# Attention and experts in one kernel: products in two parts, x taken a step later, two weight loads ahead of two stores, and ScalarE in place of GpSimd for the high parts of k

## The chip, the cores and the metric

One core of one Trainium2 chip runs one program. The metric is the device time of one execution in microseconds (us), as the median of several. Engines are named as in the profile: PE (TensorE matmul) and PEld (its weight loads), DVE (VectorE), ACT (ScalarE), POOL (GpSimd), SP (SyncE, which here issues nearly every DMA; SPq is its queue).

## The reference

Attention over 2 batches, 8 heads, 576 positions, head width 64, with a bias that a small network of the relative position gives, and then a layer of 4 experts (512 to 1024 to 512) over the 1152 rows that come out.

```python
# attention, for each batch and head
scores = (q @ k.T) / sqrt(64)
x      = log1p(|i - j|) / log1p(max(i, 1))
bias   = relu(x[..., None] @ w1 + b1) @ w2          # 32 hidden units, one bias per head
attn   = exp(scores + bias - rowmax)
attn   = attn / (sum(attn) + 1e-9)
x_attn = attn @ v
# experts
p   = domain_probs / (sum(domain_probs) + 1e-9)
out = sum over e of p[:, e] * (relu(x_attn @ W1[e]) @ W2[e])
```

## The kernel before

Matmuls whose accuracy matters are done on a high and a low part of each operand: hi is a copy of the fp32 value rounded to a shorter type, lo is the rest, and PE adds three products (hi·hi, hi·lo, lo·hi). So each operand costs two elementwise instructions ahead of PE.

The work runs in this order.

- **Bias of blocks 0 to 15** (EARLY = 16). For each block of 16 query rows DVE and ACT make the hidden layer (hidden_of_block, lines 689 to 700 and 855 to 865), PE sums it (sum_block, L988 to L1003), ACT scales it (scale_block, L867 to L874), and SP stores it to DRAM (store_rows, L480 to L483).
- **Pass 0 of attention**: the first 256 query rows, for PAIRS = 8 pairs of heads, with two steps of 128 rows for each pair. Step s of 16 is ORDER0[s] = (p, t); from step 4 on, step 2p is (p, 0) and step 2p + 1 is (p, 1). For a step PE makes scores (score_step, L1031), DVE adds the bias and takes the row maximum (add_bias, L723), ACT makes exponentials (exponents, L890), DVE inverts the sums (invert, L735 and L738), POOL scales the rows (normalise, L647), PE transposes them two steps later (turn, L1060 and L1064; LAG = 2), and ACT (turns 0, 2 and 4 of a pair) and DVE (turns 1 and 3) copy the transposed blocks out (take_turn, L896 and L743). There are two transposition banks; a turn waits until the turn two before it has been copied out. When both steps of a pair are transposed, PE multiplies by v (products, L1089; 20 matmuls), at the steps that PRODUCTS_AT names: step 5 for pair 0, 6 for pair 1, 2p + 4 for pairs 2 to 6. ACT and DVE then take the result x out in a high and a low part (high_of_x L901, low_of_x L748), in the same step and behind that step's take_turn. All x of pass 0 go through one PSUM bank, x_bank.
- **q and k**: POOL also makes the high and low parts of each pair's k and q (high_of_qk L619 and L623 in odd steps, low_of_qk L633 and L637 in even ones), three pairs ahead. SP reloads qk_raw when they are done.
- **The turn to the experts**: behind pass 0, PE runs hidden_part(0, 0), the last turns, hidden_part(0, 1), the products of pair 7, sum_block(16), hidden_part(0, 2) and sum_block(17). Of these hidden parts three of four contraction slices run at once, the last one after x of pair 7 is there. Then a table of positions (POS = 16 for each expert) weaves experts and the rest: hidden_part(0, 3) at position 3, then sum_block(18) and (19), and so on; the bias blocks 18 to 35 lie at positions 3 to 11.
- **Weights**: 64 chunks of 512 KB. Chunk n goes into w_raw slot n % 2 (load_chunk, L489 to L501, which waits until chunk n - 2 has its low part), ACT makes its high part (high_of_chunk, L912) and DVE its low part (low_of_chunk, L754). Chunks 0 and 1 are loaded in pass 0. At position 0, 1 and 2 of the first expert each of ACT and DVE first takes the hidden bank (L919, L761) and then chunk 2, 3 and 4; **at position 2 both make the hidden layer of bias blocks 18 and 19 behind chunk 4.** SP's list there is: store_rows(16), store_rows(17), load_chunk(2), load_chunk(3), and at position 0 load_chunk(4).
- **Pass 1 of attention** (the other 320 rows) is woven into the experts of the first half of the rows, and experts over the second half follow.

Every engine runs its own fixed list in order; semaphores tie them together. The order of the lists above is written out by hand.

Of the kernel before, what the change touches and what calls it, by code (L numbers as in the profile page):

```python
# [24 lines left out]
JT = 5  # L25
# [28 lines left out]
LAG = 2  # L54

# [12 lines left out]
PRODUCTS_AT = {5: 0, 6: 1, **{2 * p + 4: p for p in range(2, PAIRS - 1)}}  # L68
# [129 lines left out]
def bank_place(n):  # L198

    if n < WOVEN_FROM:  # L200
        return (3, 0, 1)[n % 3]
    if n < WOVEN_END:
        return 2 + n % 2
    return n % 4
# [6 lines left out]
def attention_and_experts(nc, qk_t, v, b_w, probs_in, w1, w2,  # L211
# [3 lines left out]
    with ExitStack() as top:  # L215
# [70 lines left out]
        qk_split, scored, maxed, exped = (sem(s) for s in ("qk_split", "scored", "maxed", "exped"))  # L286
        plus_eps, recip_done, normed = (sem(s) for s in ("plus_eps", "recip_done", "normed"))
# [39 lines left out]
        def split_count(g):  # L327

            return SPLITS[0] * min(g + 1, PAIRS) + SPLITS[1] * max(0, g + 1 - PAIRS)
# [45 lines left out]
        def x_place(f):  # L375

            if f == 0:
                return x_bank[:, 0:ROWS0].rearrange("p (c q) -> p c q", c=2)
            return score_bank[0][:, :, HALF:HALF + ROWS1 // 2]
# [42 lines left out]
        def free_bank(eng, n):  # L422

            if n < 3:
                eng.wait_ge(maxed, blk(0, PAIRS - 1, 3) + 1)
            if n == WOVEN_FROM:
                eng.wait_ge(x_lo_out, PAIRS)
            if n >= WOVEN_END and bank_place(n) < 2 and n < WOVEN_END + 4:
                eng.wait_ge(maxed, blk(1, PAIRS - 1, 4) + 1)
            if bank_before(n) is not None:  # L430
                bank_taken(eng, bank_before(n))

        with nc.Block() as block:

            @block.sync
            def _(sp):
# [85 lines left out]
                for p in range(PAIRS):  # L522
# [10 lines left out]
                    if p == 6:  # L533
                        sp.dma_start(p_raw[:, 0:2, :], probs_in[0:ROWS0, :].rearrange("(t p) e -> p t e", p=P)
                                     ).then_inc(p_in, 16)
                        sp.dma_start(p_raw[:, 2:4, :], probs_in[S:S + ROWS0, :].rearrange(
                            "(t p) e -> p t e", p=P)).then_inc(p_in, 16)
                        sp.dma_start(p_raw[:, 4:6, :], probs_in[ROWS0:4 * P, :].rearrange(
                            "(t p) e -> p t e", p=P)).then_inc(p_in, 16)
                        sp.dma_start(p_raw[0:D, 6, :], probs_in[4 * P:S, :]).then_inc(p_in, 16)  # L540
                        sp.dma_start(p_raw[D:P, 6, :], probs_in[S + ROWS0:S + ROWS0 + D, :]).then_inc(p_in, 16)
                        sp.dma_start(p_raw[:, 7:9, :], probs_in[S + ROWS0 + D:N, :].rearrange(
                            "(t p) e -> p t e", p=P)).then_inc(p_in, 16)
                store_rows(EARLY)
                store_rows(EARLY + 1)
                load_chunk(2)
                load_chunk(3)
# [49 lines left out]
            def _(pool):  # L597
# [14 lines left out]
                def high_of_qk(g):  # L612
# [6 lines left out]
                    pool.tensor_scalar(kh, k_raw, 1.0, 1.0, ALU.mult, ALU.mult).then_inc(qk_split, 1)  # L619
# [8 lines left out]
                def low_of_qk(g):  # L628
# [3 lines left out]
                    pool.wait_ge(qk_split, split_count(g) - len(pieces) - 1)  # L632
                    pool.tensor_tensor(kl, k_raw, kh.bitcast(F32), ALU.subtract).then_inc(qk_split, 1)  # L633
# [40 lines left out]
            def _(dve):  # L674
# [70 lines left out]
                def low_of_x(f, p):  # L745
                    n = PAIRS * f + p
                    dve.wait_ge(x_hi_out, n + 1)
                    dve.tensor_tensor(x_slice(x_lo, f, p), x_place(f), x_slice(x_hi, f, p).bitcast(F32),  # L748
# [29 lines left out]
                for s in range(STEPS + LAG):  # L778
# [4 lines left out]
                    if 1 <= s <= STEPS:  # L783
                        invert(0, *ORDER0[s - 1])
                    if s >= LAG:
                        p, t = ORDER0[s - LAG]
                        take_turn(0, p, 2 * t + 1)
                    if s in PRODUCTS_AT:
                        low_of_x(0, PRODUCTS_AT[s])
                    if s == STEPS - 1:  # L790
                        low_of_chunk(0)
                    if s == STEPS:
                        hidden_of_block(EARLY)
                        low_of_chunk(1)
                hidden_of_block(EARLY + 1)
# [52 lines left out]
            def _(act):  # L848
# [43 lines left out]

                def take_turn(f, p, i):
# [4 lines left out]
                def high_of_x(f, p):  # L898
                    n = PAIRS * f + p
                    act.wait_ge(weighed, n + 1)  # L900
                    act.copy(x_slice(x_hi, f, p), x_place(f)).then_inc(x_hi_out, 1)  # L901
# [19 lines left out]
                for s in range(STEPS + LAG):  # L921
# [3 lines left out]
                    if s < STEPS:  # L925
                        q, u = ORDER0[s]
                        exponents(0, q, 2 * u)
                        exponents(0, q, 2 * u + 1)
                    if s >= LAG and t == 1:
                        take_turn(0, p, 4)  # L930
                    if s in PRODUCTS_AT:
                        high_of_x(0, PRODUCTS_AT[s])
                    if s == STEPS - 1:
                        high_of_chunk(0)
                    if s == STEPS:
                        hidden_of_block(EARLY)
                        high_of_chunk(1)
                hidden_of_block(EARLY + 1)
# [48 lines left out]
            def _(pe):  # L987
# [24 lines left out]
                def score_step(f, p, t):  # L1012
# [5 lines left out]
                    elif f == 1 and p == 0 and t == 0:  # L1018
                        pe.wait_ge(scaled, BLOCKS)
                        for n in range(WOVEN_FROM - 2, WOVEN_FROM):  # L1020
# [49 lines left out]
                def products(f, p):  # L1070
# [5 lines left out]
                    if n >= 1:  # L1076
                        pe.wait_ge(x_lo_out, n)
# [5 lines left out]
                    to = x_place(f)  # L1083
                    for c in range(chunks):
                        for t in range(JT):
                            for side in range(2):
                                half = slice(D * side, D * side + D)
                                dst = x_bank[half, 0:width] if f == 0 else to[half, c, :]
# [3 lines left out]
                    mm.then_inc(weighed, 1)  # L1092
# [44 lines left out]
                for s in range(STEPS + 1):  # L1137
# [6 lines left out]
                    if s in PRODUCTS_AT:  # L1144
                        products(0, PRODUCTS_AT[s])

# [88 lines left out]
```

## Time and profile before

| what | value |
|---|---|
| median of 3 runs | 620.22 us (620.11 to 623.03) |
| the profiled execution, own time | 620.98 us |
| its span in the trace | 619.2 us |
| PE busy | 578.6 us (93%) |
| DVE, ACT, POOL busy | 295.3, 263.4, 121.7 us |
| DMA | 72.72 MB, mean 117 GB/s |
| mean granted PE clock | 0.978 of full |

Busy time is the sum of an engine's instructions without overlaps. The span is about 1.8 us shorter than the execution's own time. The chain of work that ended last is 83% PE. A row of the timeline gives start, duration, engine, line, operation, tiles, how many instructions were merged, and in brackets how long the engine had been idle before and who ended that.

### The profile page before, as it was taken

To read this page: it belongs to the slowest core of one execution; us is meant where nothing else is said; L and a number is where in the kernel's file an instruction comes from. 1 tells how busy PE (TensorE), PEld (TensorE's weight loads), DVE (VectorE), ACT (ScalarE), POOL (GpSimd) and SP (SyncE) were. 2 spreads that over 40 slices of the span, in tenths; PEclk is the share of its full clock that TensorE was granted. 3 is DMA by queue.
4 is the path that set the end of the run, shared out by engine and by line. 5 is a ranking of instruction groups with operands and counts; after the bars stand their busy time and mean duration, and the time that the engine had idled before them with its cause. 6 is when DMAs were issued, how large, how long until landed. Compare 5 with 4: busy or idle time off the path is not lost.

```text
span 619.2 us, 9781 instructions
## 1 busy us (share of the span) xinstructions
PE 578.6 (93%) x3864; PEld 466.7 (75%) x3864; DVE 295.3 (48%) x608; ACT 263.4 (43%) x506; POOL 121.7 (20%) x176
## 2 busy tenths in 40 slices
PE   3857998949999999999999999999999999999997
PEld 1345666526677888878878788998899889989986
DVE  7935667377646633464245624261255226224511
ACT  4845666357535644464336534352045015303400
POOL 5136689000001141324313331000000000000000
PEclk9868999969999999999999999999999999999999
DMA  5882565357355552173164301241223114221201
GB/s 153 227 308 79 168 196 140 107 154 223 115 168 171 171 147 92 44 238 122 47 179 125 124 35 53 85 154 34 69 73 131 35 34 137 69 69 52 85 35 51
DMA packets 60654, 72.72 MB, mean 117 GB/s; under 512 B 23232, under 2 KB 39872, under 8 KB 60608
## 3 DMA queue, kind: packets, MB, share of 16 engines
q1 hardware_dynamic: 60416, 72.08, 38.3%
q8 instruction: 31, 0.51, 0.3%
q14 instruction: 15, 0.12, 0.1%
q10 hardware_dynamic: 192, 0.01, 0.0%
HBM read 59.10 MB, written 12.98 MB: 116 GB/s over the span
## 4 chain that ended last, share of the span: by engine, by line
PE 83%; DVE 4%; DMA 4%; ACT 4%; issue 2%; POOL 2%; ACTq 0%; DVEq 0%; SPq 0%; POOLq 0%
PE m_bank L1126 12%; PE scores L1109 11%; PE x_bank L1126 11%; PE scores L1126 10%; PE m_bank L1109 9%; PE x_bank L1109 9%; PE turn L1060 4%; PE scores L1031 4%; PE scores L1089 4%; PE x_bank L1089 3%; PE scores L999 3%; PE turn L999 2%; POOL probs L647 2%; DVE hidden L699 2%; ACT w_hi L912 1%
## 5 line engine op out<-in xcount | busy, mean ns | idle before, releaser
L647 POOL TENSOR_SCALAR probs<-probs,recip 128x576 f32<-128x576 f32 x72 | 53.0, 746 | 242.8 <-DVE recip L738 242.5
L754 DVE TENSOR_TENSOR w_lo<-w_raw,w_hi 128x1024 fp32r<-128x1024 f32 x64 | 79.8, 1246 | 29.8 <-ACT w_hi L912 29.8
L723 DVE CUSTOM_DVE_ANT_0 probs<-scores,bias 128x576 f32<-128x576 f32 x72 | 52.0, 755 | 47.7 <-PE scores L1031 33.8
L896 ACT COPY probs_t<-turn 128x512 f32<-128x512 f32 (+2 forms) x80 | 42.4, 552 | 69.7 <-PE turn L1060 68.5
L912 ACT CAST w_hi<-w_raw 128x1024 fp32r<-128x1024 f32 x64 | 66.5, 1046 | 7.3 <-DMA w_raw<-w_in 7.3
L890 ACT ACTIVATE probs<-probs,neg_max 128x576 f32<-128x576 f32 x72 | 55.4, 772 | 27.4 <-DVE neg_max L723 27.3
L1060 PE MATMUL turn<-ident,probs 128*128 128x128 f32 x288 | 45.2, 286 | 5.2 <-POOL probs L647 5.0
L1109 PE MATMUL scores<-x_hi,w_hi 128*128 128x384 f32 (+2 forms) x148 | 47.9, 324 | 0.0
L1109 PE MATMUL scores<-x_lo,w_hi 128*128 128x384 f32 (+2 forms) x148 | 47.3, 320 | 0.0
L1109 PE MATMUL scores<-x_hi,w_lo 128*128 128x384 f32 (+2 forms) x148 | 47.3, 319 | 0.0
L1109 PE MATMUL m_bank<-x_hi,w_hi 128*128 128x512 f32 (+2 forms) x124 | 44.7, 361 | 0.2 <-DVE h_lo L761 0.2
L1060 PEld LDWEIGHTS turn<-ident,probs 128*128 128x128 f32 x288 | 32.9, 143 | 15.1 <-POOL probs L647 9.2
L1109 PE MATMUL m_bank<-x_hi,w_lo 128*128 128x512 f32 (+2 forms) x124 | 43.3, 349 | 0.0
L1109 PE MATMUL m_bank<-x_lo,w_hi 128*128 128x512 f32 (+2 forms) x124 | 43.1, 348 | 0.0
L919 ACT ACTIVATE h_hi<-scores 128x384 fp32r<-128x384 f32 (+2 forms) x37 | 15.3, 414 | 58.1 <-PE scores L1109 58.1
L1109 PE MATMUL x_bank<-x_hi,w_hi 128*128 128x512 f32 (+2 forms) x112 | 39.6, 353 | 0.0
L1126 PE MATMUL m_bank<-w_hi,h_hi 128*128 128x512 f32 x96 | 39.0, 406 | 0.0
L919 ACT ACTIVATE h_hi<-x_bank 128x512 fp32r<-128x512 f32 (+2 forms) x28 | 13.3, 477 | 59.9 <-PE x_bank L1109 59.9
L1109 PE MATMUL x_bank<-x_lo,w_hi 128*128 128x512 f32 (+2 forms) x112 | 38.5, 344 | 0.0
L1109 PE MATMUL x_bank<-x_hi,w_lo 128*128 128x512 f32 (+2 forms) x112 | 38.5, 344 | 0.0
L1126 PE MATMUL m_bank<-w_hi,h_lo 128*128 128x512 f32 x96 | 37.6, 391 | 0.0
L1126 PE MATMUL m_bank<-w_lo,h_hi 128*128 128x512 f32 x96 | 37.5, 390 | 0.0
(138 smaller groups left out, 1243.3 us busy)
## 6 DMA issues: line engine op xcount, KB each, us to landing
w_raw<-w_in SPq DMA_DIRECT2D x64, 512.0 KB, 3.7
qk_raw<-qk_t_in SPq DMA_DIRECT2D x16, 576.0 KB, 4.7
bias<-bias_scratch SPq DMA_DIRECT2D x16, 576.0 KB, 4.9
v<-v_in SPq DMA_DIRECT2D x32, 128.0 KB, 3.6
bias_scratch<-probs SPq DMA_DIRECT2D x13, 288.0 KB, 4.2
bias_scratch<-probs_t SPq DMA_DIRECT2D x10, 288.0 KB, 3.0
bias_scratch<-rows SPq DMA_DIRECT2D x8, 288.0 KB, 4.5
out_dram<-acc SPq DMA_DIRECT2D x8, 256.0 KB, 2.0
```

Source lines behind the costliest of these rows:

```text
L647: pool.tensor_scalar(tile, tile, recip[:, stat(f, p, j)], 1.0, ALU.mult, ALU.mult).then_inc(normed, 1)
L723: dve.tensor_tensor_reduce(probs_of(f, p, j).rearrange("p (c j) -> p c j", c=2), score_of(f, j)[:, :, 0:HALF], bias_of(f, p, j).rearrange( ...
L754: dve.tensor_tensor(lo, raw, hi.bitcast(F32), ALU.subtract).then_inc(w_lo_out, 1)
L890: act.activation(tile, tile, ACT.Exp, scale=-1.0, bias=neg_max[:, stat(f, p, j)], accum_out=row_sum[:, stat(f, p, j)]).then_inc(exped, 1)
L896: act.copy(sub_out(f, p, i), sub_in(n, i)).then_inc(out_act, 1)
L912: act.copy(hi, raw).then_inc(w_hi_out, 1)
L919: act.activation(hi, bank[:, cols], ACT.Relu).then_inc(hidden_hi, 1)
L999: mm = pe.matmul(sum_bank(n)[C * quad:C * quad + C, c, 0:HALF], w2_block[:, :, :].rearrange("p g h -> p (g h)"), hidden(n, quad)[:, HALF * ...
L1060: mm = pe.transpose(bank[:, P * t:P * t + P], probs_of(f, p, j)[:, P * t:P * t + P], ident[:, :])
L1089: mm = pe.matmul(dst, v_sb[:, 2 * (n % 2) + side, t, :], probs_t_of(f, p)[:, side, t, cols * c:cols * c + cols], start=t == 0, stop=t == J ...
L1109: mm = pe.matmul(m_bank(n)[:, 0:width], w, x, start=k == 0 and part == 0, stop=k == MT - 1 and part == 2)
L1126: mm = pe.matmul(m_bank(n), h, w[:, ft, :], start=ft == 0 and part == 0, stop=ft == FT - 1 and part == 2)
```

## The change

- PRODUCTS_AT now gives parts. For pairs 2 to 5 the products of contraction tiles 0 to 2 (12 matmuls) run in step 2p + 4 and those of tiles 3 and 4 (8 matmuls) in step 2p + 5. Pair 1 is split over steps 6 and 7. Pair 0 (step 5) and pair 6 (now at s = 16) run both parts together.
- x is taken out one step after the last part (X_AT). In DVE's list low_of_x stands ahead of that step's take_turn, in ACT's list high_of_x stands behind the exponentials and ahead of the copy of turn 4. Two PSUM banks take turns for x (last_bank for even pairs, x_bank for odd ones), so products wait for the x of the pair before the previous one; the order in which hidden and output tiles take banks is rotated.
- For pairs 3 to 7 (ON_ACT) the high part of k is an ACT copy in odd steps 3, 5, 7, 9 and 11, behind the exponentials and ahead of turn 4's copy; POOL's low part waits for it (k_high).
- SP's list has load_chunk(2) and load_chunk(3) ahead of store_rows(16) and store_rows(17).
- Chunk 0 is split at s = 16 and chunk 1 at s = 17, both before the hidden layer of blocks 16 and 17 and behind the turns of those steps. Before, chunk 0 was at s = 15, and chunk 1 at s = 16.

```diff
+ON_ACT = range(3, PAIRS)
...
-PRODUCTS_AT = {5: 0, 6: 1, **{2 * p + 4: p for p in range(2, PAIRS - 1)}}
+
+PART_T = ((0, 3), (3, JT))
+PRODUCTS_AT = {5: [(0, 0), (0, 1)], 6: [(1, 0)], 7: [(1, 1)],
+               **{2 * p + 4 + part: [(p, part)] for p in range(2, PAIRS - 2) for part in range(2)},
+               STEPS: [(PAIRS - 2, 0), (PAIRS - 2, 1)]}
+X_AT = {s + 1: p for s, parts in PRODUCTS_AT.items() for p, part in parts if part == 1}
...
-        return (3, 0, 1)[n % 3]
+        return (0, 1, 3)[n % 3]
...
-            return SPLITS[0] * min(g + 1, PAIRS) + SPLITS[1] * max(0, g + 1 - PAIRS)
+            return sum((SPLITS[o >= PAIRS]) - (o in ON_ACT) for o in range(g + 1))
...
-        def x_place(f):
+        def x_place(f, p):
 
             if f == 0:
-                return x_bank[:, 0:ROWS0].rearrange("p (c q) -> p c q", c=2)
+                return (last_bank, x_bank)[p % 2][:, 0:ROWS0].rearrange("p (c q) -> p c q", c=2)
...
+            if n == 2:
+                eng.wait_ge(x_lo_out, PAIRS - 1)
...
+                load_chunk(2)
+                load_chunk(3)
                 store_rows(EARLY)
                 store_rows(EARLY + 1)
-                load_chunk(2)
-                load_chunk(3)
...
-                    pool.tensor_scalar(kh, k_raw, 1.0, 1.0, ALU.mult, ALU.mult).then_inc(qk_split, 1)
+                    if g not in ON_ACT:
+                        pool.tensor_scalar(kh, k_raw, 1.0, 1.0, ALU.mult, ALU.mult).then_inc(qk_split, 1)
...
+                    if g in ON_ACT:
+                        pool.wait_ge(k_high, g - ON_ACT[0] + 1)
...
+                    if s in X_AT:
+                        low_of_x(0, X_AT[s])
                     if s >= LAG:
                         p, t = ORDER0[s - LAG]
                         take_turn(0, p, 2 * t + 1)
-                    if s in PRODUCTS_AT:
-                        low_of_x(0, PRODUCTS_AT[s])
-                    if s == STEPS - 1:
-                        low_of_chunk(0)
-                    if s == STEPS:
-                        hidden_of_block(EARLY)
-                        low_of_chunk(1)
-                hidden_of_block(EARLY + 1)
+                    if s >= STEPS:
+                        low_of_chunk(s - STEPS)
+                        hidden_of_block(EARLY + s - STEPS)
...
+                def high_of_k(g):
+                    act.wait_ge(raw_in[g % 2], 16 * (g // 2 + 1))
+                    act.wait_ge(scored, last_block_of(before_in_place(g)) + 1)
+                    act.copy(k_of(g)[0], qk_raw[:, g % 2, 1, :]).then_inc(k_high, 1)
...
+                    if s in X_AT:
+                        high_of_x(0, X_AT[s])
+                    if s % 2 and 3 + (s - 3) // 2 in ON_ACT:
+                        high_of_k(3 + (s - 3) // 2)
                     if s >= LAG and t == 1:
                         take_turn(0, p, 4)
-                    if s in PRODUCTS_AT:
-                        high_of_x(0, PRODUCTS_AT[s])
-                    if s == STEPS - 1:
-                        high_of_chunk(0)
-                    if s == STEPS:
-                        hidden_of_block(EARLY)
-                        high_of_chunk(1)
-                hidden_of_block(EARLY + 1)
+                    if s >= STEPS:
+                        high_of_chunk(s - STEPS)
+                        hidden_of_block(EARLY + s - STEPS)
...
-                def products(f, p):
+                def products(f, p, part=None):
+
                     n = PAIRS * f + p
                     on_act, on_dve = taken_by(f, p)
                     pe.wait_ge(out_act, on_act)
                     pe.wait_ge(out_dve, on_dve)
                     pe.wait_ge(v_in[n % 2], 48 * (n // 2 + 1))
-                    if n >= 1:
-                        pe.wait_ge(x_lo_out, n)
+                    if n >= 2:
+                        pe.wait_ge(x_lo_out, n if f else n - 1)
+                    first_t, end_t = (0, JT) if part is None else PART_T[part]
...
-                        for t in range(JT):
+                        for t in range(first_t, end_t):
                             for side in range(2):
                                 half = slice(D * side, D * side + D)
-                                dst = x_bank[half, 0:width] if f == 0 else to[half, c, :]
+                                dst = to[half, :, :] if f == 0 else to[half, c, :]
                                 mm = pe.matmul(dst, v_sb[:, 2 * (n % 2) + side, t, :],
                                                probs_t_of(f, p)[:, side, t, cols * c:cols * c + cols],
                                                start=t == 0, stop=t == JT - 1)
-                    mm.then_inc(weighed, 1)
+                    if end_t == JT:
+                        mm.then_inc(weighed, 1)
...
+                    for p, part in PRODUCTS_AT.get(s, ()):
+                        products(0, p, part)
```

## Rows read from the trace of the kernel before

**Rows 1.** The page: span, busy by engine, and one group (mean ns behind busy us).

```profile
span 619.2 us, 9781 instructions
PE 578.6 (93%) x3864; PEld 466.7 (75%) x3864; DVE 295.3 (48%) x608; ACT 263.4 (43%) x506; POOL 121.7 (20%) x176
...
L890 ACT ACTIVATE probs<-probs,neg_max 128x576 f32<-128x576 f32 x72 | 55.4, 772 | 27.4 <-DVE neg_max L723 27.3
```

**Rows 2.** What PE waited for, 38 to 142 us: total, times, longest.

```profile
PE scores L999 <- DVE probs L699: 9.7, 1, 9.7
...
PE turn L1064 <- ACT probs_t L896: 2.0, 6, 0.3
```

**Rows 3.** The chain that ended last, 104 to 136 us: start, duration, what.

```profile
107.62 0.60 PE turn L1064 x4
...
112.60 1.11 PE scores L999 x16
...
115.97 1.15 PE turn L999 x16
...
118.51 4.03 DMA w_raw<-w_in
...
124.89 3.57 DMA w_raw<-w_in
...
128.48 1.05 ACT w_hi L912
...
130.79 1.30 DVE probs L699 x3
...
132.22 2.15 PE scores L999 x16
134.37 1.79 PE turn L999 x16
```

**Rows 4.** Windows of 1 us: engines' busy time (instructions), granted clock, DMA.

```profile
49.00:50.00 1.00, 0.00 (x0) 0.00 (x0) 0.97 (x5) 1.00 (x4) 0.12 (x1) 1.00 0.00 0
...
122.00:123.00 1.00, 0.57 (x3) 0.15 (x1) 0.00 (x0) 0.44 (x1) 0.00 (x0) 1.00 0.94 365
...
125.00:126.00 1.00, 0.00 (x0) 0.00 (x0) 1.00 (x2) 0.88 (x2) 0.00 (x0) 0.83 0.03 10
...
135.00:136.00 1.00, 1.00 (x12) 0.22 (x4) 1.00 (x4) 0.17 (x1) 0.00 (x0) 0.55 0.00 0
```

**Rows 5.** The timeline, 98 to 119 us: all engines.

```profile
100.45 1.38 PE L1060 MATMUL turn<-ident,probs 128*128 128x128 f32 x8 [1.02 <-POOL probs L647]
...
101.66 1.23 DVE L754 TENSOR_TENSOR w_lo<-w_raw,w_hi 128x1024 fp32r<-128x1024 f32 x1 [1.68 <-ACT w_hi L912]
...
104.93 3.23 DVE L699 TENSOR_SCALAR probs<-table,shift 128x576 f32<-128x576 f32 x3
...
118.10 0.60 ACT L919 ACTIVATE h_hi<-m_bank 128x512 fp32r<-128x512 f32 x1 [0.21 <-PE m_bank L1109]
```

**Rows 6.** The timeline, 74 to 79.3 us: steps 9 and 10 of pass 0.

```profile
74.09 0.37 ACT L901 CAST x_hi<-x_bank 128x256 fp32r<-128x256 f32 x1 [0.86 <-PE x_bank L1089]
...
74.96 1.09 PE L1060 MATMUL turn<-ident,probs 128*128 128x128 f32 x8
...
77.67 0.57 ACT L896 COPY probs_t<-turn 64x512 f32<-64x512 f32 x1
...
77.90 1.32 PE L1060 MATMUL turn<-ident,probs 128*128 128x128 f32 x8
...
78.48 0.67 POOL L619 TENSOR_SCALAR k_hi<-qk_raw 128x576 fp32r<-128x576 f32 x1
...
78.56 0.42 PEld L1060 LDWEIGHTS turn<-ident,probs 128*128 128x128 f32 x4 [0.24 <-POOL probs L647]
```

**Rows 7.** The chain that ended last, 66 to 84 us: one pair of pass 0.

```profile
71.73 2.31 PE x_bank L1089 x20
...
79.22 2.31 PE x_bank L1089 x20
```

More of the change, by code:

```diff
@@ L286, in attention_and_experts @@
         qk_split, scored, maxed, exped = (sem(s) for s in ("qk_split", "scored", "maxed", "exped"))
+        k_high = sem("k_high")
         plus_eps, recip_done, normed = (sem(s) for s in ("plus_eps", "recip_done", "normed"))
@@ L747, in low_of_x @@
                     dve.wait_ge(x_hi_out, n + 1)
-                    dve.tensor_tensor(x_slice(x_lo, f, p), x_place(f), x_slice(x_hi, f, p).bitcast(F32),
+                    dve.tensor_tensor(x_slice(x_lo, f, p), x_place(f, p), x_slice(x_hi, f, p).bitcast(F32),
                                       ALU.subtract).then_inc(x_lo_out, 1)
@@ L900, in high_of_x @@
                     act.wait_ge(weighed, n + 1)
-                    act.copy(x_slice(x_hi, f, p), x_place(f)).then_inc(x_hi_out, 1)
+                    act.copy(x_slice(x_hi, f, p), x_place(f, p)).then_inc(x_hi_out, 1)
                 def high_of_chunk(n):
@@ L1019, in score_step @@
                         pe.wait_ge(scaled, BLOCKS)
-                        for n in range(WOVEN_FROM - 2, WOVEN_FROM):
+                        for n in range(WOVEN_FROM - 3, WOVEN_FROM):
                             bank_taken(pe, n)
@@ L1082, in products @@
                     cols = width // chunks
-                    to = x_place(f)
+                    to = x_place(f, p)
                     for c in range(chunks):
-                        for t in range(JT):
+                        for t in range(first_t, end_t):
                             for side in range(2):
                                 half = slice(D * side, D * side + D)
-                                dst = x_bank[half, 0:width] if f == 0 else to[half, c, :]
+                                dst = to[half, :, :] if f == 0 else to[half, c, :]
                                 mm = pe.matmul(dst, v_sb[:, 2 * (n % 2) + side, t, :],
@@ L1143, in _ @@
                         turns_of_step(*ORDER0[s - LAG])
-                    if s in PRODUCTS_AT:
-                        products(0, PRODUCTS_AT[s])
+                    for p, part in PRODUCTS_AT.get(s, ()):
+                        products(0, p, part)
                 def slot(at):
```

## Prediction

> **What bounds the kernel now.** I read four views, in this order. The page says that PE is busy for 578.6 of 619.2 us, so at most some 40 us lie outside its matmuls, and a change to the order of lists can only win there [rows 1]. The waits of PE in the stretch that the change touches say where: one single wait of 9.7 us ahead of sum_block(18), for the hidden layer that DVE makes at L699. Beside it the waits inside the pairs of pass 0 are small, 2.0 us in all for turn 4, which waits for the copy of turn 2 [rows 2]. The chain that ended last shows what stands in front of the 9.7 us: the load of chunk 2 is issued at 118.51, behind the second of two stores, lands at 122.54, its low part is done at 124.87, only then chunk 4 is issued, lands at 128.46, is split into high part (1.05) and low part until 130.79, and then DVE makes the hidden layer (1.30) and PE starts again at 132.22 [rows 3]. The windows of 1 us show the second price of the wait: PE's last work ends at about 122.57, its granted clock falls from full (2.4 GHz) to half (1.2 GHz) at about 125.7, 3.1 us later, and rises again at about 135.9, some 3.7 us after PE is back [rows 4].
>
> **The two loads ahead of the two stores.** This is the large term. load_chunk(2) waits for chunk 0's low part alone, which before is done at 102.9 [rows 5], so the load can be issued some 15 us earlier, at about 104, and lands by 108. load_chunk(3) waits for chunk 1's low part, which I put at 111 below; the stores behind it wait for ACT's scaling of block 16, which can't come before its sum ends at 113.7 [rows 3], so the queue is free for them and the move past them costs nothing. That cover is 2.7 us wide; a later chunk 1 would hold back both stores, which nobody near needs.
> With chunk 2 present, ACT takes it as soon as it has taken the first hidden bank: 118.10 + 0.60 [rows 5] + 1.05 for the cast [rows 3] + 0.02 + 1.23 for DVE's low part [rows 5] = 121.00, where it was 124.87. Chunk 4 is issued then, and everything behind it keeps its length: 3.57 load, 1.05, 1.23, 1.30 hidden layer [rows 3, 5]. DVE's other work there (the second and third hidden bank, as wide as ACT's copy of 0.60 [rows 5], and chunk 3's 1.23) fits into the 4.6 us between 121.0 and 125.6, since chunk 3 has landed by 115. So sum_block(18) starts 3.9 us earlier, at 128.3, and the wait is 5.8 us and not 9.7. What is late next is chunk 4 itself, because its slot is free only when chunk 2 is split. Bounds: the load took 3.57 once and 4.03 once [rows 3], so -3.9 or -3.4. Everything behind 132 is one engine's work in order and moves along: chunks 5 and 6 shift by the same 3.9 us.
>
> **The clock behind the wait.** The two sums behind it take 2.15 + 1.79 = 3.94 us at half clock; the same two sums take 1.11 + 1.15 = 2.26 us at full clock [rows 3]. The low clock costs 1.7 us. With 5.8 us without work and a fall seen 3.1 us after the stop I expect it to fall again and to cost the same: 0. A wait of about 1.7 us around 49 left it at full clock [rows 4], so the bounds are -1.7 (it stays high) and +1.7 (the low stretch is twice as long).
>
> **Pass 0, the pairs.** PE does the same matmuls in another order. An even step loses 8 of the 20 products to the odd step behind it; 20 take 2.31 us [rows 7], so 0.92 us moves. The wait of turn 4 for the copy of turn 2 stays (the turns stand next to each other as before). What can be won: in even steps from 8 on the second turn waits for POOL's row scaling, so that 8 transpositions take 1.32 us, against 1.09 in odd steps [rows 6]: 0.23 us in each of 4 steps, 0.9 us in all. With 0.92 us more work between odd scores and the even step's turns, POOL is ready in time, and that wait goes. What is late next is ACT. The second turn of an even step needs the copy of turn 4, which before ended at 78.24, 0.33 us ahead of 78.56 where that turn ran [rows 6]. Now the products give it 0.92 us more, and it is set back by the k copy and by DVE, whose turn copy now stands behind x. The k copy on ACT does not exist in the trace; 128x576 exponentials take 0.77 [rows 1] and the 128x1024 cast 1.05 [rows 3], a 64x512 copy 0.57 [rows 6]. I take 0.67, nearest to the row of equal width without its bias and sum. DVE: x comes behind two exponentials and ACT's 0.37 copy [rows 6]; by my laying out of the step, DVE reaches the next odd scores 0.5 us late. Slack: 0.33 + 0.92 - 0.67 - 0.5 = 0.1 us, about what there was for POOL. So in the three even steps behind a k copy (8, 10, 12) nothing is won, and in step 14 some 0.2 us. Bounds: -0.9 (all four) and +1.3 (k copy 1.0 us, three to four times).
> GpSimd loses 0.67 us per pair for pairs 3 to 7 [rows 6]. It has that slack in the middle of the pass, so this alone is worth 0 there. In the turns of pair 7 PE does wait for it, 1.02 us at 100.45 [rows 5]; the pairs there (8, 9) keep their k on POOL, and it starts that stretch about 0.3 us earlier.
>
> **The end of pass 0.** Chunk 0 is split one step later. ACT must copy turn (7, 0), copy x of pair 5 and cast chunk 0 (about 0.6 + 0.37 + 1.05), then DVE needs 1.23: together 3.25 us behind the first turn, against 0.66 for the second turn and 2.31 for the products [rows 7] on PE, 2.97. So of the 0.3 to 0.5 us by which that turn comes earlier, hidden_part(0, 0) keeps about 0.1 to 0.2. Chunk 1 is cast behind turn 4's copy of pair 7: 107.62 + 0.60 [rows 3] + 0.57 + 1.05 + 1.23 = 111.1; hidden_part(0, 2), which needs it, runs at 113.7. The wait for last_bank and the rotated banks hit free banks. Sum for all of pass 0: -0.2 us, with bounds -1.0 and +1.7.
> A row shows one danger here: three DVE instructions at 104.93 took 3.23 us beside POOL's work, while three of the same shape take 1.30 with POOL idle [rows 5, 3]. Chunk 0's low part took 1.23 at 101.66 [rows 5] and now falls at about 102.8, beside POOL's row scaling. The Trainium skill ("SBUF — State Buffer", section "Who interferes with whom") has a rule that speaks against the move: a VectorE instruction with two SBUF inputs and a GpSimd instruction that reads SBUF share one port pair, and the one that is issued second fully blocks. By that rule chunk 0's low part could stand behind one scaling of 0.73 us and hidden_part(0, 0) would start about 0.4 us later, and the sum would end at 616.5. The 3.23 us agree with it.
>
> **The sum.** -3.9 (load), 0 (clock), -0.2 (pass 0) = -4.1 us. The profiled execution took 620.98 us, so its counterpart would take 616.9 with a span of 615.1. The median of the runs, 620.22, is 0.76 below that one execution; the same 4.1 us off it gives 616.1.
>
> **The rivals.**
> 1. The clock stays high, because the wait is 4 us shorter. For it: 1.7 us at 49 didn't lower it [rows 4]. Against: 5.8 us is well over the 3.1 us after which it fell. It gives 616.1 - 1.7 = 614.4.
> 2. The clock comes back later, after some 7 us and not 3.7: 616.1 + 1.7 = 617.8.
> 3. Pass 0 wins its full 0.9 us and the earlier turn of pair 7 holds: 616.1 - 0.7 - 0.3 = 615.1.
> 4. The loads aren't early, or something else ends the wait at 132 (the change doesn't do what it says). For it: DVE's order at position 2 is unchanged, hidden layer behind chunk 4. Against: every link of the chain back to the store is a load or a split of a chunk [rows 3]. It gives 620.22 - 0.2 = 620.0.
> 5. On the other side: ACT sets the pace of pass 0. The place is a pair's odd step, where k copy (0.67), x copy (0.37) and DVE's x (0.42) all stand in one ring, scores to exponentials to x to the turn copy to the next scores. Where they lie in series and nothing hides them, each of the 5 pairs gains 1.46 us, 7.3 in all: 616.1 + 7.3 = 623.4. It decides against the change from 0.8 us per pair on, since 5 x 0.8 uses up the 4.1. Against it: a pair takes 7.49 us (79.22 - 71.73) [rows 7], ACT's work for one is 4 x 0.77 + 3 x 0.57 + 0.37 + 0.67 = 5.8, and it sat idle for 0.86 us ahead of x alone [rows 6].
>
> **How the numbers follow.** Forecast 616.1: 0.60. Rival 1: 0.14. Rival 2: 0.07. Rival 3: 0.08. Rival 4: 0.06. Rival 5: 0.05. A measurement of this kernel tells about 0.5% (3.1 us) from no change. Faster by over that (below 617.1) are rivals 1 and 3 and the forecast but for some 0.05 at its late end: 0.77. Within: rivals 2 and 4, that 0.05 and part of rival 5, 0.19. Slower: 0.04. The range takes in rivals 1 and 3 and the forecast's own bounds (load +0.5, pass 0 +1.7) and reaches to rival 2: 613.8 to 618.4.
>
> **What the next profile shows.** The large term is right if chunk 2's load is issued at about 104, ACT's cast of it stands directly behind the first hidden bank's copy, chunk 4 is issued near 121 and sum_block(18) waits under 6 us. It is wrong if PE's wait there still is 9 us. The clock term is read in the windows behind it: half clock for 3 to 4 us more of work. The term of pass 0 is right if a pair still takes about 7.5 us and an even step's 8 transpositions take 1.1 to 1.3 us; if turns wait for ACT's copy of turn 4 by more than 0.3 us each, rival 5 has come in part. The forecast falls if PE waits for more than 3 us in all behind 140 us, where now it is busy nearly throughout.

## The result and the profile after

| what | before | after |
|---|---|---|
| median | 622.55 us (7 runs, 620.11 to 623.26) | 618.31 us (7 runs, 617.07 to 619.85) |
| ratio to before | | 0.9945 (0.993 to 0.996) |
| profiled execution, own time / span | 620.98 / 619.2 us | 618.14 / 616.3 us |
| PE's wait ahead of sum_block(18) | 9.65 us | 5.91 us |
| PE, DVE, ACT, POOL busy | 578.6, 295.3, 263.4, 121.7 us | 580.0, 295.9, 265.9, 117.9 us |

The change makes the kernel 0.55% faster, with 0.4 to 0.7% in the interval. The kernel before ran in seven runs at a median of 622.55, not at the 620.22 of the three shown ahead of the prediction. The ratio is that of the means of the seven runs each, 618.50 and 621.92 us, and it is the number to go by; the two medians are a little further apart (4.2 us against 3.4).

The waits of PE in the changed kernel, 38 to 142 us (engine, line, who was waited for: total, times, longest). They answer to [rows 2].

```profile
...
PE scores L1012 <- DVE probs L711: 5.9, 1, 5.9
...
PE scores L1125 <- DVE w_lo L766: 0.7, 1, 0.7
PE turn L1077 <- ACT probs_t L910: 0.3, 1, 0.3
...
PE turn L1073 <- DVE probs_t L755: 0.2, 1, 0.2
```

The first of these lines is the 9.7 us of before, now 5.9. Two lines are new: 0.7 us for chunk 0's low part, and a small wait for DVE's copy of a turn. The wait of turn 4 for ACT, 2.0 us in six parts before, is down to one; the run with the turn copy ahead of x shows below what took its place.

The chain that ended last in the changed kernel, 118 to 133 us (start, duration, what), against [rows 3]:

```profile
118.42 0.60 ACT h_hi L933
119.02 0.94 ACT w_hi L926
...
119.99 1.24 DVE w_lo L766
...
121.24 3.80 DMA w_raw<-w_in
...
125.06 1.05 ACT w_hi L926
...
126.14 1.23 DVE w_lo L766
127.37 1.30 DVE probs L711 x3
...
128.80 2.15 PE scores L1012 x16
130.95 1.92 PE turn L1012 x16
```

Chunk 2's load, issued at 104.29 in this trace, and the store ahead of it are gone from the chain. ACT casts the chunk directly behind the first hidden bank, chunk 4 is issued at 121.24, and the rest is as long as before but for the load (3.80 us, where it took 3.57).

The windows of 1 us behind it (PE, PEld, DVE, ACT, POOL busy, granted clock, DMA share, GB/s), against [rows 4]:

```profile
122.00:123.00 1.00, 0.89 (x4) 0.39 (x3) 1.00 (x2) 0.00 (x0) 0.00 (x0) 1.00 0.42 113
...
126.00:127.00 1.00, 0.00 (x0) 0.00 (x0) 0.86 (x1) 1.00 (x3) 0.00 (x0) 1.00 0.97 375
127.00:128.00 1.00, 0.00 (x0) 0.00 (x0) 1.00 (x3) 1.00 (x3) 0.00 (x0) 0.53 0.03 12
...
133.00:134.00 1.00, 1.00 (x3) 0.81 (x4) 1.00 (x3) 1.00 (x2) 0.00 (x0) 0.56 0.90 223
```

PE stopped at 122.9, the clock fell to half at about 127.1 and rose at about 133.9. PE worked for 5.1 us at half clock, where before it was 3.7 us. The wait is shorter, the slow stretch of work behind it is longer.

### The profile page after: what moved, and what is told of

It reads as the page before. It is cut to its first block, busy times and chain, and to the rows that moved or that the text cites. A ratio compares the mean times of both kernels' runs of the same rounds, so it can differ in the third digit from the quotient of the medians.

```text
span 616.3 us, 9802 instructions
## 1 busy us (share of the span) xinstructions
PE 580.0 (94%) x3864; PEld 466.2 (76%) x3864; DVE 295.9 (48%) x608; ACT 265.9 (43%) x511; POOL 117.9 (19%) x171
## 4 chain that ended last, share of the span: by engine, by line
PE 81%; ACT 5%; DVE 5%; DMA 3%; issue 3%; POOL 2%; ACTq 0%; DVEq 0%; POOLq 0%
PE m_bank L1142 12%; PE scores L1125 12%; PE x_bank L1142 11%; PE scores L1142 10%; PE m_bank L1125 9%; PE x_bank L1125 9%; PE turn L1073 4%; PE scores L1104 4%; PE scores L1044 3%; PE scores L1012 3%; PE turn L1012 2%; ACT probs L899 1%; POOL probs L659 1%; ACT w_hi L926 1%; DVE w_lo L766 1%
## 5 line engine op out<-in xcount | busy, mean ns | idle before, releaser
L1125 PE MATMUL scores<-x_hi,w_hi 128*128 128x256 f32 (+2 forms) x152 | 50.0, 329 | 0.9 <-DVE w_lo L766 0.7
L1125 PE MATMUL scores<-x_lo,w_hi 128*128 128x256 f32 (+2 forms) x152 | 49.1, 323 | 0.0
L1125 PE MATMUL scores<-x_hi,w_lo 128*128 128x256 f32 (+2 forms) x152 | 48.9, 322 | 0.0
L1125 PE MATMUL m_bank<-x_hi,w_hi 128*128 128x512 f32 (+2 forms) x120 | 42.9, 358 | 0.0
L1125 PE MATMUL m_bank<-x_hi,w_lo 128*128 128x512 f32 (+2 forms) x120 | 41.7, 347 | 0.0
L1125 PE MATMUL m_bank<-x_lo,w_hi 128*128 128x512 f32 (+2 forms) x120 | 41.6, 346 | 0.0
```

The costliest lines, as they stand in the source:

```text
L1125: mm = pe.matmul(m_bank(n)[:, 0:width], w, x, start=k == 0 and part == 0, stop=k == MT - 1 and part == 2)
```

## The experiments

All ratios are to the kernel before, with 95% intervals. Five rounds each, but for the early chunk 0 with three. The changed kernel's own is 0.9945 (0.993 to 0.996).

A second measure helps where the traces differ early on. From the start of sum_block(17) (115.97 in [rows 3], 116.29 in the changed kernel's trace) to the end of the span it is 503.2 us in the kernel before and 500.0 in the changed one.

**The loads alone.** The kernel before with one edit:

```diff
+                load_chunk(2)
+                load_chunk(3)
                 store_rows(EARLY)
                 store_rows(EARLY + 1)
-                load_chunk(2)
-                load_chunk(3)
```

> The kernel before with one edit: the loads of chunks 2 and 3 ahead of the stores of blocks 16 and 17. My theory (the load order carries the whole gain): PE's wait ahead of sum_block(18) falls from 9.7 to about 5.8 us, and the time by 3.4 to 4.4 us against before, ratio 0.993 to 0.9945, as much as the full change. Rival (the parts in pass 0 are worth something of their own, or the early load collides with other transfers): the ratio stays above 0.996.

Ratio 0.993 (0.9905 to 0.9955), median 618.45 us. The chain that ended last in that kernel:

```profile
121.03 1.24 DVE w_lo L754
...
122.28 3.54 DMA w_raw<-w_in
...
129.58 2.15 PE scores L999 x16
```

It has the same links as the changed kernel's, and PE's wait is 5.64 us. From sum_block(17) to the end it is 499.5 us. The load order gives the whole gain; the interval holds the changed kernel's ratio.

**The loads late again.** The changed kernel with that one edit undone.

> The changed kernel with the loads of chunks 2 and 3 behind the two stores again. My theory: the wait ahead of sum_block(18) is 9.5 us again; what is left against before is pass 0 alone, 0 to -1 us, ratio 0.9985 to 1.0. Rival (pass 0 is worth more than 1 us): ratio below 0.998.

Ratio 1.0017 (0.9999 to 1.0034). The wait ahead of sum_block(18) is 9.66 us again, and from sum_block(17) to the end it is 502.9 us. Everything else in the change together wins nothing, and may cost 1 us. Both halves of the same question agree.

**k on GpSimd.**

```diff
-ON_ACT = range(3, PAIRS)
+ON_ACT = range(0)
```

> The changed kernel with the high part of k on GpSimd for all pairs. My theory for pass 0 (ACT's copy of turn 4, set back by the k copy, stands ahead of the second turn of even steps): with k on GpSimd the pair is not longer than 7.42 us, and the kernel is within 0.5 us of the changed one. Rival (GpSimd paced the turns, and k on ACT frees them): pairs take 7.5 us again and the second turn waits for GpSimd, 0.1 to 0.2 us per pair, some 0.5 to 1 us slower than the changed kernel.

Ratio 0.9932 (0.9907 to 0.9957), the same as the changed kernel. In the trace a pair takes 7.42 us (scores at 71.57, 79.00 and 86.41), as with k on ACT (7.41). ACT against GpSimd is worth nothing here. My bound for it was right and the reason was not: the k copy stands beside the path, not on it: the chain of the changed kernel, shown with the next run, has no k copy in it.

**The products undivided.** The changed kernel with the products of pairs 1 to 5 in one step, x still a step later.

```diff
-PRODUCTS_AT = {5: [(0, 0), (0, 1)], 6: [(1, 0)], 7: [(1, 1)],
-               **{2 * p + 4 + part: [(p, part)] for p in range(2, PAIRS - 2) for part in range(2)},
+PRODUCTS_AT = {5: [(0, 0), (0, 1)], 6: [(1, 0), (1, 1)],
+               **{2 * p + 4: [(p, 0), (p, 1)] for p in range(2, PAIRS - 2)},
```

> The changed kernel with the products of pairs 1 to 5 undivided again, in the step of their first part; x is still taken a step later. My theory (the split moves 0.92 us of PE work in front of the even step's turns and by that gives GpSimd's scaling the time it lacked): without it the second turn of even steps waits again for GpSimd or ACT, some 0.2 to 0.9 us per pair, 1 to 3 us slower than the changed kernel in all, and x, being taken behind the exponentials, sets DVE back as well. Rival (the split does nothing): the same time within 0.5 us.

Ratio 1.0031 (1.0012 to 1.0049), 624.65 us: slower than before, in spite of the early loads, and 6 us above the changed kernel. That is more than the 1 to 3 us I gave it. One pair of its pass 0, from the chain that ended last:

```profile
70.47 0.98 PE scores L1044 x11
71.45 0.60 PE turn L1073 x4
...
72.07 0.59 ACT probs_t L910
...
73.23 0.95 ACT probs L899 x3
74.18 0.27 ACT x_hi L915
...
74.47 0.07 DVE x_lo L760
...
74.81 0.69 DVE probs_t L755
...
75.64 1.06 PE turn L1073 x8
76.70 2.31 PE m_bank L1104 x20
79.01 0.99 PE scores L1044 x12
```

A pair takes 8.54 us (79.01 - 70.47). PE waits 1.25 us ahead of turn 0 of four pairs (2.24 ahead of a fifth), since DVE copies the pair before's turn 3 only when x is out, and x stands behind ACT's exponentials. So a ring like that of rival 5 exists. The ring of the same links, one step later (turn 0 to turn 3), stands in the changed kernel's chain:

```profile
77.90 0.60 PE turn L1073 x4
...
78.52 0.59 ACT probs_t L910
79.11 1.52 ACT probs L899 x4
80.63 0.27 ACT x_hi L915
...
80.92 0.42 DVE x_lo L760
81.34 0.61 DVE probs_t L755
...
82.09 0.63 PE turn L1073 x4
...
84.32 0.99 PE scores L1044 x12
```

It takes as long as there, 4.19 us from the first turn to the turn that waits (77.90 to 82.09, and 71.45 to 75.64). But a pair's scores start at 76.91 and the next pair's at 84.32, 7.41 us later, because here twelve products run on PE while the ring turns:

```profile
78.85 1.51 PE L1104 MATMUL x_bank<-probs_t,v 128*64 128x256 f32 x12
```

With the products whole, x falls into the odd step, which has no products to fill that time. So the split pays back what the later x costs; whether whole products with x taken in an even step would do as well was not run. That the rest of my expectation, a wait for GpSimd, would return did not happen: PE waits for DVE.

**The turn copy ahead of x.** The changed kernel with two lines swapped in DVE's list: take_turn first, low_of_x behind it.

> The changed kernel with DVE's turn copy ahead of its low part of x. My theory now (a pair of pass 0 takes 7.41 us because of the ring turn 0, ACT's copy, two exponentials, x high, x low, DVE's copy of turn 1, turn 3): the copy no longer waits for x, turns 3 wait no longer for DVE, and a pair takes 7.2 to 7.3 us; 0.5 to 0.9 us faster than the changed kernel in the trace, which the timing can hardly tell. Rival (the ring isn't what sets the pair, PE's own work is): 7.41 us again.

Ratio 0.9943 (0.9924 to 0.9963), no difference. The ring is gone from the chain, and a pair still takes 7.40 us. One pair of it:

```profile
77.34 0.99 PE scores L1044 x12
78.33 1.02 PE turn L1073 x8
79.36 1.45 PE x_bank L1104 x12
80.80 0.99 PE scores L1044 x12
81.79 0.60 PE turn L1073 x4
...
82.42 0.59 ACT probs_t L910
...
83.14 0.60 PE turn L1077 x4
83.74 1.01 PE x_bank L1104 x8
84.76 0.99 PE scores L1044 x12
```

My theory that the ring alone sets the 7.41 us fell, and the time is the rival's; but PE's own work does not fill it, since turn 4 waits 0.33 us a pair for ACT's copy of turn 2 again (2.0 us in six parts, as before). In the changed kernel turn 3 waits as long for DVE's copy of turn 1: its odd step's eight transpositions take 1.43 us and not 1.09, and turn 4 then waits for nothing. One wait stands in for the other. What the pair does win, 7.41 against 7.49 us, is on PE's list: the even step's transpositions take 1.09 us and not 1.32 [rows 6], and of these 0.23 us 0.15 goes into the split, since the 20 products in two parts take 1.45 + 1.01 = 2.46 us against 2.31 whole [rows 7].

**x in the step of its products.** The changed kernel, x taken behind the turn copies of the same step.

```diff
-X_AT = {s + 1: p for
+X_AT = {s: p for
```

> The changed kernel with x taken in the step of the last part of its products, behind the turn copies, as the kernel before did it. My theory: nothing waits for x, so a pair takes 7.2 to 7.3 us like the kernel with the turn copy ahead of x; the delay of x is not needed, once the products are in two parts. Rival (taking x right behind the products holds ACT and DVE up ahead of the next scores): 7.5 us or more.

Ratio 0.9993 (0.9979 to 1.0007). The pairs take 7.41 us (76.31 to 83.72), so here too the expectation of 7.2 to 7.3 was wrong. But the kernel loses its gain at the end of pass 0: x of pair 6 now stands in ACT's list ahead of chunk 0's cast, which starts at 103.42, and PE waits 2.8 us for chunk 0's low part (0.7 in the changed kernel). Its clock falls there as well: the first matmul behind the wait takes 0.71 us, and from there to sum_block(16) PE needs 10.0 us (105.90 to 115.91) against 8.4 (104.41 to 112.85). The 2.1 us of wait and the 1.6 us behind it cover the loss: sum_block(16) starts 3.1 us later than in the changed kernel, and from sum_block(17) to the end both take the same (499.9 and 500.0 us). The later x is needed there, not in the pairs.

**Chunk 0 one step earlier.** The changed kernel, chunk 0 split at step 15.

> The changed kernel with chunk 0 split one step earlier again (step 15). My theory: in the changed kernel PE waits 0.7 us ahead of hidden_part(0, 0), since chunk 0's low part starts late and took 1.64 us beside GpSimd's scaling and not 1.23; split at step 15 it takes 1.23 and that wait is gone. 0.3 to 0.7 us faster than the changed kernel. Rival (that wait only hides another, GpSimd's scaling of pair 7): wait gone, the next turns wait instead, time the same within 0.2 us.

Ratio 0.9936 (0.9909 to 0.9964). The wait of 0.7 us is gone and the low part takes 1.23 us again; the timing can't tell it from no difference. The rows of the two kernels, first the changed one (its POOL row gives the shortest, median and longest of two in ns, and when the first and the last began):

```profile
L659 POOL TENSOR_SCALAR probs<-probs,recip x2: 747/1226/1704, 102.4 to 103.2; 128x576 f32<-128x576 f32 x2
...
102.56 1.71 DVE L766 TENSOR_TENSOR w_lo<-w_raw,w_hi 128x1024 fp32r<-128x1024 f32 x1
```

and the one with chunk 0 early:

```profile
102.27 1.23 DVE L766 TENSOR_TENSOR w_lo<-w_raw,w_hi 128x1024 fp32r<-128x1024 f32 x1 [1.40 <-ACT w_hi L929]
102.38 1.65 POOL L629 TENSOR_SCALAR k_hi<-qk_raw 128x576 fp32r<-128x576 f32 x1
```

An instruction grew where it began while the other engine's was under way. In the changed kernel GpSimd's first scaling, begun at 102.45, takes 0.75 us, DVE's low part, begun 0.1 us behind it, 1.71 and not 1.23, and GpSimd's second scaling, begun within that, 1.70. With chunk 0 early DVE's begins first and takes 1.23, and GpSimd's k copy takes 1.65 where it took 0.67 [rows 6].

**Fillers in the wait.** The changed kernel with work on PE that nobody reads; its outputs lie in a bank that sum_block(18) writes over.

```diff
+                        if ge == 0 and pos == 3:
+                            pe.wait_ge(scaled, EARLY + 1)
+                            for _ in range(36):
+                                pe.transpose(score_bank[0][:, 0, 0:P], ident[:, :], ident[:, :])
                         if ge == 0 and pos in BIAS_AT:
```

> The changed kernel with 36 transpositions of the identity that nobody reads, on PE in the wait ahead of sum_block(18), about 5 us of work. My theory (the fall of the clock behind the wait costs 2.4 us: 5.1 us of work at half clock): the clock stays at full in 122 to 134, the two sums take 2.3 us and not 4.1, and the time falls by 1.8 to 2.6 us against the changed kernel. Rival (what counts there is DVE, ACT or the loads, so PE would only wait later): clock full, but new waits of PE in 131 to 140 us and a gain under 0.7 us.

Ratio 0.9931 (0.991 to 0.9952), median 617.1. The granted clock stays at full (2.4 GHz):

```profile
127.00:128.00 1.00, 0.00 (x0) 0.00 (x0) 1.00 (x4) 0.38 (x2) 0.00 (x0) 1.00 0.23 78
128.00:129.00 1.00, 0.82 (x16) 0.50 (x16) 1.00 (x4) 0.97 (x1) 0.00 (x0) 1.00 1.03 354
```

From the start of sum_block(18) to the end of the span it is 613.6 - 128.18 = 485.4 us, in the changed kernel 616.3 - 128.80 = 487.5. That prices the slow stretch at 2.1 us in the trace. The ratios, 0.9931 and 0.9945, differ by 0.9 us and their intervals overlap: the price is seen in the trace, the timing does not settle it.

**The hidden layer ahead of chunk 4.** The changed kernel with hidden_of_block(18) and (19) ahead of the chunk at position 2, for DVE and ACT.

> The changed kernel with the hidden layer of bias blocks 18 and 19 ahead of chunk 4 in DVE's and ACT's lists. My theory (chunk 4's load is what the hidden layer waits for, without needing it): sum_block(18) starts at about 125.2 and not 128.8; then hidden_part(0, 4) waits for chunk 4's low part, which DVE has about 128.5. PE idles 5.9 us before and about 2 + 1.5 us now, and the clock may stay at full: 2 to 4.5 us faster than the changed kernel. Rival: the split of chunk 4 is late by as much as the sums are early, under 1 us.

Ratio 0.9902 (0.9876 to 0.9929), 614.89 us. PE's wait ahead of sum_block(18) is 2.1 us. Behind it the chain that ended last runs over chunk 5: it lands at 129.15, ACT casts it and only then scales blocks 18 and 19, and PE goes on with block 20 at 132.92. The clock fell here too, at about 126.2, 2.4 us after PE had stopped and when it was already back, and stayed at half for 3.4 us. But PE waits only 0.2 us ahead of block 20, so this slow stretch lies beside the chain over chunk 5.

**The hidden layer earliest.** The changed kernel with the hidden layers of 18 and 19 ahead of the first hidden bank (DVE), and for ACT between the two scalings and ahead of chunk 3.

> The changed kernel with the hidden layer of bias blocks 18 and 19 made before the first hidden bank is taken, in DVE's idle 4.3 us ahead of 119 (ACT: block 18 between two scalings, block 19 ahead of chunk 3). My theory: no wait ahead of sum_block(18), PE goes on at 122.9 to about 125, and then hidden_part(0, 4) waits for chunk 4's low part, ready at about 127.4: one wait of 2.4 us, no fall of the clock. 3.5 us less wait and 2.4 us less at half clock: 5 to 6 us faster than the changed kernel, ratio to before 0.983 to 0.986. Rival (the chain of chunk 4, 5, 6 sets the time from here on): the win stops at 3.5 us.

Ratio 0.9908 (0.989 to 0.9926), 616.19 us. No wait ahead of sum_block(18) is left and the one ahead of hidden_part(0, 4) is 2.4 us, as expected, but the ratio is above what I gave. Part of the chain:

```profile
129.35 4.55 PE scores L1130 x12
133.91 1.11 PE scores L1017 x16
...
135.99 2.94 PE m_bank L1130 x12
```

The clock fell behind 2.4 us of idling too, at about 129.3, and the first hidden part took 4.55 us where the next took 2.94, a loss of 1.6 us. I had counted on full clock. In the trace it is 495.7 us from sum_block(17) to the end, 4.4 less than in the changed kernel, and not 5 to 6. That full clock would have given the rest is not so: the next kernel has it here and takes as long.

**All three.** The last kernel with chunk 0 split at step 15 and the turn copy ahead of x.

> The kernel with the hidden layer of blocks 18 and 19 made earliest, and with chunk 0 split at step 15 and DVE's turn copy ahead of x. My theory: the waits of 0.7 us (chunk 0) and of 5.9 us are gone, one of 2.4 us for chunk 4 stays; against the kernel before the ratio is 0.987 to 0.990, some 6 to 8 us. Rival: the clock falls in or behind the 2.4 us as it did there, and the ratio is 0.990 or above.

Ratio 0.9877 (0.9855 to 0.9899), 614.61 us, as expected: the lowest median here, though its interval overlaps those of the two runs before. In its profile the wait for chunk 4 is 2.3 us and the clock stays at full from 118 to 146. Yet from sum_block(17) to the end it takes 495.7 us, the same as the kernel before it with 1.6 us lost to the clock. What the clock gives back, PE now waits for ahead of sum_block(20) (from its waits, 38 to 150 us, and the chain):

```profile
PE scores L1023 <- ACT bias L878: 1.4, 1, 1.4
...
132.89 1.18 PE scores L1023 x16
```

That is 15.3 us behind the start of sum_block(17), against 15.6 in the kernel before it (133.91 - 118.35) and 15.7 with the hidden layer ahead of chunk 4. The chain there runs over chunk 5, its cast on ACT and ACT's work for blocks 18 to 21. So the rival of the run before, the chain of the chunks sets the time from here on, holds in kind. Work of no use in the wait of 2.3 us was not measured.

**Two edits on the kernel before.** The loads ahead of the stores and the hidden layer earliest, nothing of pass 0.

```diff
                 dve.wait_ge(p_steps, 3 + E)
+                hidden_of_block(EARLY + 2)
+                hidden_of_block(EARLY + 3)
...
                 scale_block(EARLY)
+                hidden_of_block(EARLY + 2)
                 scale_block(EARLY + 1)
```

> The kernel before with two edits only: the loads of chunks 2 and 3 ahead of the stores, and the hidden layer of bias blocks 18 and 19 made ahead of the first hidden bank. Nothing of pass 0 is changed. My theory (pass 0's four edits are worth nothing, the chain of chunks 2 and 4 is all there is): ratio to before 0.987 to 0.991, as the kernel with all three. Rival (the edits of pass 0 carry 1 us or more of it, which the load order alone could not show): ratio above 0.991.

Ratio 0.9885 (0.9864 to 0.9905), 615.18 us; 496.2 us from sum_block(17) to the end. It can't be told from the kernel with all three, with none of the edits of pass 0. The wait of PE that is left at this place (from its waits, 38 to 150 us):

```profile
PE scores L1114 <- DVE w_lo L754: 2.3, 1, 2.3
```

The wait of 9.7 us for the hidden layer is gone, and one of 2.3 us for chunk 4's low part has come in its place.

## Why the prediction was right or wrong

**What bounds the kernel, and the load term: right.** The forecast was -3.9 us, PE's wait 5.8 us, chunk 4 issued near 121. Measured: 5.91 us and 121.24. Against ACT's first hidden bank, which came 0.32 us later in this trace (118.42, 118.10 in [rows 5]), sum_block(18) moved by 3.42 + 0.32 = 3.7 us. The 0.2 us that are missing are chunk 4's load, 3.80 and not 3.57 us, inside the bound that I gave. The single edit, alone and undone, shows that this is the cause: behind sum_block(17) the two kernels with late loads take 503.2 and 502.9 us, and the two with early loads 500.0 and 499.5.

**The clock: the direction right, the size missed.** It fell again, as forecast, but I put the difference at 0, with 1.7 us to either side. PE worked 5.1 us at half clock and not 3.7, which is 0.7 us more. That term was 0 in the sum and measured 0.7; it lies between the forecast and rival 2. Rival 1 did not come in. What spoke for rival 1, the 1.7 us at 49 that left the clock at full, was one row: in the same profile the clock fell near 57.4, 2.0 us after PE had come back from a wait of 1.77.

**Pass 0: the sum about right, the step wrong.** I gave -0.2 us. The run with the loads late gives +0.17% (-0.01 to +0.34%), some 1 us on the bad side, inside my bounds. A pair takes 7.41 and not 7.49 us, so 0.08 us is won where I had nothing in three of four even steps. The reading that failed here is "what is late next is ACT", the copy of turn 4 set back by the k copy; that copy took 0.66 us, as I took it, and costs nothing. What is late is DVE's copy of turn 1, behind x. I had that delay at 0.5 us and let it count only through the exponentials to turn 4; its direct way, to turn 3, is the one in the chain. And I did not count that the products in two parts take 0.15 us longer than whole. That the sum of pass 0 came out near is in part luck: two sizes that I had wrong are both small.

**The end of pass 0: the size right, but left out of the sum.** My working had chunk 0's low part 0.3 us behind PE (3.25 against 2.97), and another 0.4 us as the effect of GpSimd beside it, which I left out of the sum. PE waited 0.7 us there, and the low part took 0.5 us longer (1.71 against 1.23). One thing in that passage is wrong: the 3.23 us at 104.93 are of instructions with a single tensor input (TENSOR_SCALAR), so they show that DVE and GpSimd slow each other, but do not bear on a rule for two inputs. The rows of the run with chunk 0 early do.

**The sum: the difference held, the base failed.** The change itself measured 0.55% (0.4 to 0.7%), 3.4 us, against 4.1 us in the forecast, which is 0.66%, within the interval. The step of the prediction that failed is its last: "The median of the runs, 620.22, is 0.76 below that one execution; the same 4.1 us off it gives 616.1." I took a median of three runs for the kernel's own time. Seven runs of the same kernel gave 622.55, others on later chips 621.85 to 622.93, with single runs from 619.57 to 625.04. So the base was 2.3 us too low, and the profiled execution is not 0.76 us above the median but 1.6 below it. The result of 618.31 lies 2.2 us above the forecast, at the late end of the range; held against 620.22 it would look like a gain of only 1.9 us.

With 622.55 as base the same 4.1 us would have given 618.45. That this is so near to 618.31 is partly luck: by the means, 621.92 - 4.1 = 617.8 against 618.50, the sum is 0.7 us off. That is as much as the clock term had wrong, though differences of that size lie within the noise.

Where the spread comes from is seen in part. The start of the scores of step 5 (PE's last wait of 1.77 us there) lies at 55.45 in the profile before, and at 55.16, 56.71 and 57.24 in three profiles of kernels that are alike up to there (the fillers, the changed kernel, the early chunk 0): up to 2 us without any edit. In the changed kernel's profile the clock is full from 50 to 60, before it is 0.87 there. So the 2.9 us between the two profiled executions are not the change term by term: about 1.3 us of later start work against it, and a fall of the clock near 58 that only the first of the two has works for it. How much of the spread is loads and how much clock stays open.

**The rivals.** Rivals 3 and 4 did not come in: pass 0 won nothing that the timing shows, and the loads were early. **Rival 5** named a ring that exists, but not quite its links and not its condition. The k copy is not in it: it runs from a turn over ACT's copy, the exponentials and x to DVE's turn copy and the next turn. It lengthened the pairs only when the split was taken away: then it costs 1.05 us a pair (8.54 against 7.49), close to the 0.8 per pair from which I had it decide, and the kernel is slower than before.

## What to carry to other kernels

When a long wait ends in a chain of transfer, split, transfer, look in the issuing queue for the first link that stands behind something it does not need; one swap of two lines was the whole gain of a change of a hundred. Then look at the waiting work itself: the hidden layer needed no chunk at all and only stood behind one in its engine's list, which was worth as much again. A forecast for a change of half a per cent needs the spread of the base; give the difference, and take the base from many runs.

## What the runs showed of the hardware

- The granted clock fell to half (1.2 GHz) 3.1 us after PE stopped in the profile before and 4.2 us after in the changed kernel's, both within the wait. It also fell behind waits of 2.1, 2.4 and 2.3 us (hidden layer ahead of chunk 4, hidden layer earliest, two edits on the kernel before), 2.4 to 2.7 us after the stop, when PE was just coming back or had been back for up to 0.4 us; behind another wait of 2.3 us (all three) it stayed at full. So these profiles do not show a length of wait below which the clock stays at full.
- Waits of 1.7 and 1.8 us went either way: in the changed kernel's profile they left the clock at full from 50 to 60, in the profile before it fell near 57.4, 2.0 us after PE had come back.
- What the slow stretch added to the chain was 1.6 to 2.1 us in the kernel before, the changed one and the one with the hidden layer earliest, and the shorter wait of the changed kernel had a longer stretch of work at half clock (5.1 us) than the longer wait before (3.7).
- 36 transpositions of no use in a wait of 5.9 us kept the clock at full and saved 2.1 us in the trace.
- A DVE instruction with two inputs in SBUF grew from 1.23 to 1.71 us when it began 0.1 us after a GpSimd instruction, and GpSimd's k copy grew from 0.67 to 1.65 us when it began 0.1 us after DVE's. The Trainium skill ("SBUF — State Buffer", section "Who interferes with whom") has this as a lock on a port pair in which the order of issue decides who waits; these rows agree with it.
